# Router logits of six token tiles: from TensorE to GpSimd, ScalarE and VectorE in a fused attention and mixture kernel

## What is computed

```
attn_out = _attn_ref(q, k, v)
x = attn_out.transpose(0, 2, 1, 3).reshape(B * S, H * D)
xn = x / rms * rms_g
g = xn @ w_gate
silu = g * (1.0 / (1.0 + np.exp(-g)))
y = silu * (xn @ w_val) @ w_out
logits = y @ router_w + modality_bias[modality_id]
e_idx = np.argmax(logits, axis=1)
out[mask] = gate_w[mask, None] * (relu(y[mask] @ w1[e]) @ w2[e])
```

## Time and profile before

| | us |
|---|---|
| median of three runs | 872.52 |
| lowest and highest | 872.29, 872.88 |
| span of the profiled execution, first to last instruction | 870.5 |
| TensorE busy | 857.1 |
| VectorE busy | 520.7 |
| ScalarE busy | 374.4 |
| GpSimd busy | 328.4 |

### The profile page before, as it was taken

How to read it: one execution, slowest core, us unless ns; L and a number is a source line. 1 busy time by engine, 2 the same in 40 slices (tenths; PEclk the granted TensorE clock), 3 DMA queues, 4 the chain that set the end, 5 groups by cost and what they waited for, 6 DMA issues and landing times.

```text
span 870.5 us, 15612 instructions
## 1 busy us (share of the span) xinstructions
PE 857.1 (98%) x5233; PEld 736.4 (85%) x5242; DVE 520.7 (60%) x1401; ACT 374.4 (43%) x945; POOL 328.4 (38%) x372
## 2 busy tenths in 40 slices
PE   8999999999999999999999999999999999999997
PEld 5678898888888888899999999988888888888885
DVE  6985555333453335449778763883877457666663
ACT  6966313545464455443321132243356235554442
POOL 3736762344323443356335333170043221222211
PEclk9999999999999999999999999999999999999999
DMA  9983212212223210242121121526265645555531
GB/s 191 289 212 88 61 48 65 84 55 78 53 60 112 52 38 27 71 157 74 42 93 61 61 73 37 210 81 254 97 205 206 241 144 191 184 213 182 192 128 39
DMA packets 77517, 103.40 MB, mean 119 GB/s; under 512 B 38973, under 2 KB 43069, under 8 KB 77312
## 3 DMA queue, kind: packets, MB, share of 16 engines
q1 hardware_dynamic: 73760, 91.16, 33.9%
q0 software_dynamic: 3680, 11.28, 3.7%
HBM read 92.98 MB, written 10.22 MB: 119 GB/s over the span
## 4 chain that ended last, share of the span: by engine, by line
PE 89%; DVE 8%; issue 1%; ACT 1%; POOL 1%; DMA 1%; SPq 0%; DVEq 0%; POOLq 0%; ACTq 0%
PE ps L1243 32%; PE ps L1282 16%; PE ps L1805 13%; PE ps L1790 13%; PE ps L1174 3%; PE ps L1203 2%; PE ps L1815 2%; PE ps L1184 2%; PE ps L1150 2%; PE ps L660 1%; DVE sm L1520 1%; DVE w_lo L2041 1%; DMA qk<-in_k 1%; PE ps L1312 1%; DVE h_lo L1600 1%
## 5 line engine op out<-in xcount | busy, mean ns | idle before, releaser
L1035 POOL TENSOR_TENSOR sm<-sm,rinv 72x288 f32<-72x288 f32 (+1 forms) x51 | 45.5, 893 | 174.2 <-DVE rinv L1531 174.1
L1067 POOL TENSOR_TENSOR out_lo<-out_raw,out_hi 128x512 fp32r<-128x512 f32 x72 | 101.8, 1414 | 5.8
L1589 DVE SCALAR_TENSOR_TENSOR h<-h,ps 128x384 f32<-128x384 f32 x72 | 39.8, 553 | 104.2 <-ACT h L1437 103.3
L1243 PE MATMUL ps<-x_hi,val_hi 128*128 128x384 f32 x288 | 101.1, 351 | 0.0
L1243 PE MATMUL ps<-x_hi,gate_hi 128*128 128x384 f32 x288 | 100.5, 349 | 0.4 <-DVE h L1589 0.4
L1065 POOL CAST out_hi<-out_raw 128x512 fp32r<-128x512 f32 x72 | 50.0, 694 | 135.0 <-DMA out_raw<-in_moe_w_out 135.0
L1441 ACT ACTIVATE h_hi<-h 128x384 fp32r<-128x384 f32 x72 | 37.8, 525 | 138.7 <-DVE h L1595 138.7
L1243 PE MATMUL ps<-x_hi,gate_lo 128*128 128x384 f32 x288 | 97.1, 337 | 0.0
L1243 PE MATMUL ps<-x_hi,val_lo 128*128 128x384 f32 x288 | 96.6, 336 | 0.0
L1243 PE MATMUL ps<-x_lo,val_hi 128*128 128x384 f32 x288 | 96.5, 335 | 0.0
L1243 PE MATMUL ps<-x_lo,gate_hi 128*128 128x384 f32 x288 | 93.9, 336 | 0.0
(11 more groups left out here) (278 smaller groups left out, 1947.5 us busy)
## 6 DMA issues: line engine op xcount, KB each, us to landing
w_raw<-in_moe_w SPq DMA_DIRECT2D x72, 512.0 KB, 4.9
out_raw<-in_moe_w_out SPq DMA_DIRECT2D x72, 256.0 KB, 2.6
x_rows<-y_tiles SPq DMA_DIRECT2D x18, 256.0 KB, 2.7
early_w_raw<-in_moe_w SPq DMA_DIRECT2D x8, 512.0 KB, 7.6
gate_raw<-in_moe_w_gate SPq DMA_DIRECT2D x4, 768.0 KB, 9.1
val_raw<-in_moe_w_val SPq DMA_DIRECT2D x4, 768.0 KB, 10.5
qk<-in_q SPq DMA_DIRECT2D x8, 288.0 KB
qk<-in_k SPq DMA_DIRECT2D x8, 288.0 KB
```

The lines of the kernel that those rows point to most:

```text
L1035: pool.tensor_tensor(s3, s3, rinv[0:n, i, :].unsqueeze(2).to_broadcast([n, 4, c]), ALU.mult).then_inc(s_no, 1)
L1067: pool.tensor_tensor(ol[i][:, :], o_raw[i][:, :], oh[i][:, :].bitcast(f32), ALU.subtract).then_inc(s_ol, 1)
L1243: mm = pe.matmul(ps[:, bank, 0:CH], w[:, i, kk, cols], x[:, kk, :], start=(m == 0), stop=(m == n - 1))
L1589: dve.scalar_tensor_tensor(out=hf[n % 2][:, :], in0=hf[n % 2][:, :], scalar=1.0, in1=ps[:, 0, 0:CH], op0=ALU.add, op1=ALU.mult).then_inc(s ...
```

## The change

No tile is turned on TensorE before the dense layer has ended. The logits of tiles 9, 10, 11 (chunk 3) and 14 (chunk 4) are made of eight products each on GpSimd, 128x512 `ys` by a router column into one of three buffers `times` (`times_router`), which ScalarE copies in place with an accumulated sum (`add_up`); VectorE adds the bias (`add_bias_to_sums`). Tiles 12 and 13 (chunk 4) go to VectorE's `dot`, read from `ys` in place. The 72 dots on reloaded tiles end at tick 65 of chunk 4 and not in chunk 5. The products of chunk 3's tiles lie on ticks 4 to 61 of chunk 4 (24), those of tile 14 on ticks 2 to 18 of chunk 5 (8), the 16 new dots on ticks 2 to 20 of chunk 5. ScalarE's sums stand one tick behind the products. The copy of the next `y` into `ys` now waits for the products and dots. `sm_early` has a place of its own, and a wait for the router's load moves to the last tiles' logits.

```diff
-Y_TILE = {(NC - 2, t): at(NC - 1, 1 + t, 0) for t in range(TT)}
-LOGITS = {k: s + 2 for k, s in Y_TILE.items()}
...
-for c in range(NC - 3, NC - 2):
-    free = [at(c + 1, f, 1, 1) for f in range(1, FT) if at(c + 1, f, 1, 1) not in QK_AT]
-    for t in range(TT):
-        Y_TILE[c, t], LOGITS[c, t] = free[t], free[t + 1]
...
-DOTTED = TT * (NC - 3)
+RELOADED = TT * (NC - 3)
+DVE_TILES = list(range(RELOADED)) + [TT * (NC - 2), TT * (NC - 2) + 1]
+POOL_TILES = [TT * (NC - 3) + t for t in range(TT)] + [TT * (NC - 2) + 2]
+DOTTED, SUMMED = len(DVE_TILES), len(POOL_TILES)
...
-DOT_TICKS = [s for s in range(at(NC - 3, 5, 0), at(NC - 1, 1, 0, 1)) if PAUSE[1] < (s - EARLY) % SPAN < PAUSE[0]]
+AGAIN_TICKS = [s for s in range(at(NC - 3, 5, 0), at(NC - 1, 0, 0)) if PAUSE[1] < (s - EARLY) % SPAN < PAUSE[0]]
+FRESH_TICKS = list(range(at(NC - 1, 0, 1), at(NC - 1, 3, 2)))
+DOT = {**spread(AGAIN_TICKS, 0, RELOADED), **spread(FRESH_TICKS, RELOADED, DOTTED - RELOADED)}
+TIMES = {**spread(list(range(at(NC - 2, 0, 2), at(NC - 2, 10, 2))), 0, TT), **spread(FRESH_TICKS[:-1], TT, SUMMED - TT)}
...
+            def times_router(i, e):
+                n = E * i + e
+                if n == 0:
+                    pool.wait_ge(s_rwe, E)
+                    pool.wait_ge(s_ye, NC - 2)
+                if i == TT and e == 0:
+                    pool.wait_ge(s_ye, NC - 1)
+                if n >= 3:
+                    pool.wait_ge(s_sm, n - 2)
+                pool.tensor_tensor(times[n % 3][:, :], ys[:, POOL_TILES[i] % TT, :], rw_of[e][:, :],
+                                   ALU.mult).then_inc(s_tm, 1)
...
+                if c == NC - 2:
+                    act.wait_ge(s_tm, E * TT)
+                if c == NC - 1:
+                    act.wait_ge(s_dot, E * DOTTED)
+                    act.wait_ge(s_tm, E * SUMMED)
...
+            def add_up(i, e):
+                act.wait_ge(s_tm, E * i + e + 1)
+                if e == 0 and i >= 2:
+                    act.wait_ge(s_lp, i - 1)
+                act.activation(times[(E * i + e) % 3][:, :], times[(E * i + e) % 3][:, :], ACT.Copy,
+                               accum_out=sums[:, i % 2, e:e + 1]).then_inc(s_sm, 1)
...
+                y = y_again[i % 3][:, :] if again else ys[:, DVE_TILES[i] % TT, :]
...
-                    dve.wait_ge(s_le, EARLY_TILES - DOTTED)
+                    dve.wait_ge(s_lp, SUMMED)
```

More of the change, by code:

```diff
@@ L143, with spread @@
+DOTTED, SUMMED = len(DVE_TILES), len(POOL_TILES)
 ROUTER = at(NC - 3, 3, 1)
 PAUSE = (SPAN - 6, 0)
-DOT_TICKS = [s for s in range(at(NC - 3, 5, 0), at(NC - 1, 1, 0, 1)) if PAUSE[1] < (s - EARLY) % SPAN < PAUSE[0]]
-DOT = {(i, e): DOT_TICKS[(E * i + e) * len(DOT_TICKS) // (E * DOTTED)] for i in range(DOTTED) for e in range(E)}
+def spread(ticks, first, n):
+    return {(first + i, e): ticks[(E * i + e) * len(ticks) // (E * n)] for i in range(n) for e in range(E)}
+AGAIN_TICKS = [s for s in range(at(NC - 3, 5, 0), at(NC - 1, 0, 0)) if PAUSE[1] < (s - EARLY) % SPAN < PAUSE[0]]
@@ L150 @@
+SUM_AT = by_tick((k, s + 1) for k, s in TIMES.items())
+SUMMED_AT = by_tick((i, TIMES[i, E - 1] + 2) for i in range(SUMMED))
+RELOAD_AT = by_tick((i, DOT[i, 0] - 8) for i in range(RELOADED))
 BY_EXPERT_AT = by_tick((e, DOT[0, e] - 1) for e in range(E))
@@ L352, in fused_kernel @@
         dots = ra.put("dots", [P, 2, E])
+        times = [ra.put(f"y_times_router{i}", [P, DM]) for i in range(3)]
+        sums = ra.put("sums", [P, 2, E])
         re = Region(xT_at)
@@ L1353, in front_pe @@
                     spread_roots(c)
-                for key in LOGITS_AT.get(s, []):
-                    logits(*key)
-                for key in Y_AT.get(s, []):
-                    turn_y(*key)
                 if s == COUNT_1:
```

102 lines of the change are left out of this document (26 added, 76 removed).

## The result

| | before | after |
|---|---|---|
| median, us | 872.4 | 897.99 |
| lowest and highest, us (4 runs each) | 872.05, 872.88 | 895.55, 901.23 |
| span of the profiled execution, us | 870.5 | 895.8 |

The changed kernel is slower: ratio 1.0291, 95% interval 1.0272 to 1.031. The forecast had the direction and not the size: 876.1 us was forecast, at most 883.

The account below looks back on a forecast made before the run. TensorE, busy for 98% of the span, was taken to bound the kernel. 870.5 - 7.7 + 6.0 + 5.3 = 874.1 us of span, plus 2.0 for the median, gave 876.1 us; range 867 to 883.

Parts of the forecast that it names:

- 7.7 us forecast: TensorE, chunks 4 and 5: six tiles' logits and transposes removed, 1.28 us each, all on the path.
- rival (e): TensorE: the change does not take from it the 7.7 us it says; chance under 0.02.
- Nothing forecast as long as GpSimd is in time: ScalarE, chunk 4: 24 sums of 0.8 us fit and hide under TensorE; GpSimd's lateness would become ScalarE's.
- rival (b): Chunks 4 and 5: VectorE and GpSimd take turns at SBUF and that decides, slower, 874.3 to 880 us; chance 0.45.
- The signs named for it: Next profile: chunk 4 blocks 4 to 9 at 7 to 8.5 us, dots' mean above 1.2, TensorE waiting for VectorE.
- The price of a product: GpSimd, one 512-column product of two operands: bounds 1.04 and 1.29 us, 1.04 taken.
- Rival (c): GpSimd: products cost as subtractions, 1.29 us, adding 7.8 us of turns, 883.9 us; chance 0.10, above 880.
- The sum of 71.2 us: Chunk 4: turns queued before VectorE's scaling of block 10, putting the arrival at t = 72.9; 49.6 before the change.
- late by 6.0 us: Chunk 4: TensorE's gate product of block 11 waits for VectorE's scaling; late by 6.6, taken as 6.0 us.
- The slack of 3 us that the chain has is in that: Chunk 4: the chain's 3 us of slack is already counted in the 6.0 us of lateness.
- Rival (d): TensorE's clock falls in (b)'s pauses, 1 to 2 us more each, 878 to 880 us; chance 0.03, on top of (b).
- Lateness goes to the end in full: Chunk 5: 5.3 us of lateness at block 3's value product reaches TensorE's count undiminished, with no slack between.

Follow-up runs that it names:

- short dots: Changed kernel with VectorE's dots cut from 512 columns to 8, products and sums whole; chunk 4 76.6 us, against 98.28 in the change.
- products alone: Kernel before plus 24 GpSimd products in chunk 4 that nobody reads, TensorE's tile work kept; 887.3 us (before 872.5), chunk 4 95.75.
- memsets of the same length: Kernel before plus 24 GpSimd memsets of 128x1536 at the same ticks, reading nothing; 875.71 us, chunk 4 82.49.
- the forms: Kernel before plus eight unread 512-column GpSimd forms, three each, run also with dots of 8 columns: two different tiles 1.32 us, one tile twice 1.04.
- the run with squares: Changed kernel with GpSimd's products of y and a router column replaced by y times itself; chunk 4 92.10 us, chunk 5 78.27.
- The kernel with tiles 12 to 14 alone: Kernel before with only chunk 4's part of the change: 12 and 13 by dots, 14 by GpSimd, 9 to 11 on TensorE; 879.17 us, ratio 1.0088.
- tile 9 on GpSimd: Kernel with even dots (12 and 13 by VectorE) plus eight GpSimd products for tile 9 in chunk 4; 873.98 us, ratio 1.002.
- the kernel with even dots: Kernel before with tiles 12 and 13 by dots, no products, reloaded dots placed where VectorE has room; 869.36 us, ratio 0.9956.
- short products: Changed kernel with GpSimd's products and ScalarE's sums cut from 512 columns to 8, dots whole; chunk 4 76.8 us.
- halves: Kernel before with one part of the change each: chunk 3's tiles by GpSimd, 891.7 us; chunk 4's tiles by dots and GpSimd, 879.17 us.

## Why the prediction was right in kind and wrong in size

**What leaves TensorE.** 7.7 us forecast. With short dots, where TensorE waits for nobody, chunks 4 and 5 are 3.9 and 4.5 us shorter, 8.4; 0.4 of it is the one wait that the kernel before had in chunk 5. Right; rival (e) falls.

**ScalarE.** Nothing forecast as long as GpSimd is in time, and its lateness otherwise; the sums added 0.6 us of lateness where GpSimd was late. Right, with less coupling than I feared.

**Turns.** The mechanism, rival (b), is shown: products alone bring 15.3 us into chunk 4 with nobody reading them (13.0 of lateness, the rest clock), memsets of the same length 2.0, and without either partner nothing is left. The signs named for it are there, and more than named: the dots' mean is 1.22 us, and not only blocks 4 to 9 but blocks 1 to 3 of chunk 4 too are longer than 7 us (7.3, 8.2, 8.0). The Trainium skill ("SBUF — State Buffer", "Who interferes with whom") says that a VectorE instruction with two SBUF inputs contends with a GpSimd instruction that reads SBUF and not with one that only writes it; by that rule too the trace agrees, by the memsets' 1.372 to 1.388 us.

**The price of a product: the first step that failed.** I bounded it by 1.04 and 1.29 us and took the lower, since "two quite different pairs of operands lie on one line that the additions miss, which speaks for the operation and not the operands". All multiplications of before read one tile (twice, or with a repeated operand) and all additions and subtractions two; the rows couldn't separate the two readings, and the forms show that it was the operands. It is 1.32. In the change: 98.28 - 92.10 = 6.2 us in chunk 4 and 80.39 - 78.27 = 2.1 in chunk 5. Rival (c), given 0.10, had nearly this price and 883.9 us; it should have had at least a half. The Trainium skill ("GPSIMD Engine Reference", "Instruction dispatch") gives 2.5 cycles an element as a floor of two-input instructions. I set that aside for the squares' sake. By the forms a tile with itself is cheaper, 1.04 against 1.32 us, and by the prediction's own rows a column costs 1.65 ns there against 2.1; so this was no floor of all two-input instructions but a fair warning for two different tiles.

**Chunk 4, the end of the turns taken for the end of VectorE's work: the second.** The sum of 71.2 us gave the time at which GpSimd is through with its products, and I took it for VectorE's arrival at the scaling of block 10. VectorE came there 7.5 us later in the run with squares, where the product has my price: the roots and diagonals (3.8 us), the bias additions and the PSUM scalings were in no term of the sum. The wait that I named was the wrong one as well. I had TensorE late by 6.0 us at block 11's gate product, for the scaling; it was late by 13.9 us in block 10, for the diagonals, and the scaling was then in time. Before, that row stood in VectorE's idle time. "The slack of 3 us that the chain has is in that" hid this.

**The clock: the third.** Rival (d) was given 0.03 and came true in both chunks. In the profiled execution the clock stood at its lower level, 1.2 GHz, for 3.4 us in block 10 of chunk 4 and again in block 4 of chunk 5, each time from 0.6 to 0.9 us after the end of a TensorE wait of 3.1 or 3.2 us; each costs 1.7 us. Behind the wait for the diagonals (length, busy times, granted clock in the third column from the end):

```profile
520.50:524.00 3.50, 3.50 (x9) 2.61 (x10) 3.46 (x12) 0.67 (x2) 0.00 (x0) 0.59 0.02 7
```

The length of the wait alone doesn't decide. The kernel with tiles 12 to 14 alone had a wait of 3.4 us at the same count and the clock stayed full; tile 9 on GpSimd had the drop behind a wait of 1.9 us, and the run with products only had one behind a wait of 1.2 us and the small matmuls of a tile's logits. What does decide stays open. Ahead of chunk 4, where the kernels don't differ, the changed kernel's profile has another such stretch, from 46.5 to 54 us (granted clock 0.83 from 40 to 50 us, full before), which costs 3.4 us; the kernel with even dots, the fastest of all, had one too, half as long (0.84 from 40 to 50 us).

**Chunk 5.** The lateness at the value product of block 3 was forecast as 5.3 us. With squares VectorE's scaling there comes at t = 27.9, with short products, in time, at 22.6: 5.3. With the true price it is 7.3. The count is where I missed more. "Lateness goes to the end in full" is right, but TensorE's 3.8 us of tile work stood before the count, and VectorE's chain to it did not get shorter: short products, late nowhere else, wait 2.5 us there, of which 1.3 are turns with GpSimd's split. So 2.5 of what is removed in chunk 5 is no gain even with products of 8 columns.

**The sum again.** In chunk 4, 15.6 us more than forecast: 6.2 price, 7.9 VectorE's row (13.9 of lateness with squares, where 6.0 was forecast), 1.7 clock, 0.2 too much by rounding and by what left TensorE. In chunk 5, 5.2 more: 2.1 price, 1.7 clock, 1.4 that I put down to the count, though the 2.5 there and the lateness overlap and I can't divide them. Ahead of chunk 4, 2.6 more, with 3.4 of clock in it; behind chunk 5, 1.7 less, which is a stretch at the lower clock that the kernel before had there (605.5 to 609.5 us) and the changed one had not. Together 21.7, the difference of 895.8 and 874.1. The numbers for price and halves are from runs of their own; the 7.9 and the clock are read from timelines, and no run takes VectorE's row away by itself.

**The range.** It ended at 883, just under (c)'s own 883.9, and so took in neither (c) whole nor (c) with (d), and no case in which (b)'s own sum was short. (Its lower end, 867, is a fifth of the lateness and not a third, which would be 868.6.) Turns, price and clock all push one way: a late VectorE makes pauses, and pauses can cost clock.

## What to carry to other kernels

When two engines share a way to memory, neither's idle time is free: add the turns of both, then add the rest of the work of the waited-for engine, ask which of its results is waited for first, and look at the block in which it falls, not at the chunk. A price taken from rows of another form should be bounded by what the forms share, here the number of different tiles read, before the operation is believed; a run with the true form says more than the argument. And two tiles moved to places with room brought 0.4% where six tiles cost 2.9%.
